# A Fourier filter ahead of a mixture of experts: corner turns on TensorE instead of through DRAM, and the imaginary sum of each product on GpSimd

## The chip, the core and the metric

The kernel runs on one core of one Trainium2 chip. The metric is the device time of one execution in microseconds (us). Less is better. The engines are TensorE (PE; its weight loads are PEld), VectorE (DVE), ScalarE (ACT), GpSimd (POOL) and SyncE (SP), which here only issues DMAs.

## What is computed

```python
batch, seq, dim = (8, 3072, 256)
X = np.fft.rfft(x, axis=1)                       # x: 8 x 3072 x 256
y = np.fft.irfft(X * (filt_r + 1j * filt_i)[None], n=3072, axis=1)
x = y.reshape(24576, 256)                        # tokens
logits = x @ w_gate                              # 8 experts
expert_idx = np.argmax(logits, axis=1)           # top 1; gate_w: its softmax
# each expert takes its first 768 tokens, in order; later ones are dropped
h = np.maximum(np.einsum('ecd,edf->ecf', disp, w1), 0.0)   # 256 -> 1024
y = np.einsum('ecf,efd->ecd', h, w2)                       # 1024 -> 256
out[i] = gate_w[i] * y[expert_idx[i], pos[i]]    # kept tokens; the others are 0
```

## The kernel before

**Which batches.** An expert is full after 768 tokens, so the first 2.5 batches hold all tokens that count, if the draw is not odd. The program runs batches t = 0, 1, 2 (`run(0, 0, FIRST)`), of the last one only half the tokens, and behind it 16 expert blocks of 384 tokens (`BLOCKS`). A second pass over the other batches stands behind a branch and is not taken.

**The transform of a batch** of 3072 tokens, seen as 128 x 24, goes in two matmul steps each way, and between them the data must be turned, from one index on the partitions to the other.

- `pe_a`: 12 matmuls of 512 columns with `wa` (item i), out to PSUM, copied to `t_out` by ScalarE (`act_a`), written to the DRAM scratch `zt` by `t_store` (issued by ScalarE and SyncE) and read back turned by `z_load`.
- `pe_forward(t, h)`: for each of eight groups h, 16 small matmuls of `z_in` into the PSUM tile `wide`. `dve_multiply` makes the four products with the filter `fab` (two instructions of 1024 columns into `prod`), `dve_sums` the real difference and the imaginary sum into `yy`. The one `wide` tile makes the next forward wait for both multiplies (`p_done`).
- `pe_inverse(t, j)`: 16 small matmuls of `yy` with `wbi`. `act_back` copies them to `v_out` and writes the DRAM scratch `vt`; `v_load` or `v_chunk` read it turned.
- `pe_product`: 12 matmuls of 512 columns with `wai` (6 of other shape for the half batch); `act_rows` copies them to `y`, which `y_store` writes to `y_rows` in DRAM, where experts gather from.
- For the router, `pe_turn` transposes `y` (four transposes of 128x128 for each product), `act_turned` copies, `pe_logits` multiplies with `w_gate`, `pe_raw` turns the logits back. `dve_route` makes ranks and slots in 30 small steps on VectorE (the largest ones, `hot_lo`, `hot_eq`, `hot_hi`, are one-hot matrices), and `pe_table` sums them into the table of tokens.

**Order.** Each engine has its own list, written out by hand. In the stage of batch t (`pe_stage`, 16 half steps h) TensorE also does `pe_a` of batch t + 1 and the tokens (product, turn, logits, raw) of batch t - 1, which run on into the next stage. In the last stage the order is a list of its own (`pe_last_stage`), and `pe_last` has the half batch's tokens.

**Experts.** A block is gathered by GpSimd (`pool_gather`), transposed (`pe_block_turn`), split into a high and a low part (`xh`, `xl`), multiplied (`up`, 48 matmuls; `down`, 72), each in three of the four part products. Weights are split the same way: the high part by ScalarE (`act_split`), the low part by VectorE for w1 and GpSimd for w2 (`low_split`). Their tiles lie over those of the transform.

## Time and profile before

| | |
|---|---|
| three runs | 538.6, 540.87, 543.45 us (median 540.87) |
| the profiled execution | 543.3 us, span 541.3 us |
| mean granted TensorE clock | 0.942 |
| busy: PE, DVE, ACT, POOL | 460.6, 246.9, 206.0, 202.3 us |
| DMA | 117.28 MB, mean 217 GB/s |

The span runs from the first to the last instruction. The granted clock is a share of 2.4 GHz; the other level is 1.2 GHz, and a number between them is a mix of both over the stretch. The busy time of an engine is an average over stages with different limits, so it has to be read stage by stage.

### The profile page before, as it was taken

Reading aid. Unit: us, or ns where it says so; the run is one execution under the profiler, and the core shown is the slowest. Engines: PE = TensorE matmul, PEld = TensorE weight load, DVE = VectorE, ACT = ScalarE, POOL = GpSimd, SP = SyncE. Lnnn points to the kernel's source line nnn. Section 1 sums busy time; section 2 is a strip of 40 time slices with the busy share of each in tenths; the row PEclk is TensorE's granted clock in tenths of the full one; section 3 lists DMA queues with packets and bytes.
Section 4 is the critical chain, followed back from the end, with each engine's and each line's share of the span. In section 5 each row is a group of like instructions: output and inputs, shape, how many; then the busy total and the mean of one; then the engine's idle time right before and its main releaser. Section 6 shows DMA issues by size and latency. Waiting matters only on the chain.

```text
span 541.3 us, 10327 instructions
## 1 busy us (share of the span) xinstructions
PE 460.6 (85%) x4190; PEld 368.3 (68%) x4190; DVE 246.9 (46%) x381; ACT 206.0 (38%) x362; POOL 202.3 (37%) x181
## 2 busy tenths in 40 slices
PE   5454977899789757988988998999999999998994
PEld 2112323345445424477988998999999999997994
DVE  2058235465666989578716332345412534133210
ACT  2301433455345314534135533344543436333221
POOL 0140100000000000637355788655867556684222
PEclk9958878999989977988999999999999999999998
DMA  8899897998597825999513209931099130681001
GB/s 298 298 361 413 279 380 240 316 377 275 171 339 250 281 72 151 375 409 380 192 61 106 79 11 360 377 129 40 31 332 386 54 134 30 223 316 46 30 22 44
DMA packets 63224, 117.28 MB, mean 217 GB/s; under 512 B 7632, under 2 KB 35056, under 8 KB 62656
## 3 DMA queue, kind: packets, MB, share of 16 engines
q1 hardware_dynamic: 38560, 75.77, 39.0%
q0 software_dynamic: 8864, 23.46, 12.4%
q10 hardware_dynamic: 15744, 17.31, 10.1%
q8 instruction: 35, 0.57, 0.4%
q14 instruction: 21, 0.17, 0.1%
HBM read 58.29 MB, written 58.23 MB: 215 GB/s over the span
## 4 chain that ended last, share of the span: by engine, by line
PE 58%; DVE 9%; DMA 5%; issue 5%; ACT 3%; SPq 2%; ACTq 0%; POOL 0%; POOLq 0%; DVEq 0%
PE psum L1335 23%; PE psum L1321 22%; PE psum L558 3%; PE psum L519 2%; PE psum L692 2%; PE psum L503 2%; DVE prod L832 2%; DMA w_raw<-in_w 2%; SPq L399 1%; PE psum L573 1%; DMA t_scratch<-t_out 1%; DVE hot_lo L983 1%; DMA g_in<-y_rows,token 1%; DMA u_scratch<-v_out 1%; PE psum L538 1%
## 5 line engine op out<-in xcount | busy, mean ns | idle before, releaser
L1146 DVE SCALAR_TENSOR_TENSOR hl<-psum,hh 128x384 fp32r<-128x384 f32 x128 | 69.0, 555 | 150.5 <-ACT hh L1098 113.5
L1335 PE MATMUL psum<-w2h,hh 128*128 128x256 f32 x384 | 109.8, 286 | 0.0
L1335 PE MATMUL psum<-w2h,hl 128*128 128x256 f32 x384 | 108.6, 283 | 0.0
L1335 PE MATMUL psum<-w2l,hh 128*128 128x256 f32 x384 | 108.6, 283 | 0.0
L832 DVE TENSOR_TENSOR prod<-psum,fab 128x1024 f32<-128x1024 f32 x48 | 56.5, 1219 | 90.8 <-PE psum L503 58.1
L1321 PE MATMUL psum<-xh,w1h 128*128 128x384 f32 x256 | 88.0, 344 | 9.6 <-DVE hl L1146 5.0
L1098 ACT ACTIVATE hh<-psum 128x384 fp32r<-128x384 f32 x128 | 60.7, 492 | 72.4 <-PE psum L1321 55.9
L1321 PE MATMUL psum<-xh,w1l 128*128 128x384 f32 x256 | 86.9, 339 | 0.0
L1321 PE MATMUL psum<-xl,w1h 128*128 128x384 f32 x256 | 86.8, 339 | 0.0
L1235 POOL DMA_INDIRECT out<-o_out,token x48 | 50.6, 1054 | 84.5 <-ACT o_out L1107 66.8
L1335 PEld LDWEIGHTS psum<-w2h,hh 128*128 128x128 f32 x384 | 73.6, 192 | 0.2 <-issue 0.2
L1335 PEld LDWEIGHTS psum<-w2l,hh 128*128 128x128 f32 x384 | 73.6, 192 | 0.0
L1335 PEld LDWEIGHTS psum<-w2h,hl 128*128 128x128 f32 x384 | 73.6, 192 | 0.0
L1207 POOL DMA_INDIRECT g_in<-y_rows,token x48 | 52.4, 1093 | 36.9 <-DVE token L1017 21.1
L1107 ACT ACTIVATE o_out<-psum,o_gate 128x256 f32<-128x256 f32 x48 | 22.8, 475 | 102.4 <-PE psum L1335 100.0
L1219 POOL DMA_INDIRECT o_gate<-gate_rows,token x48 | 48.7, 1014 | 23.6 <-issue 14.4
L1321 PEld LDWEIGHTS psum<-xh,w1h 128*128 128x128 f32 x256 | 49.1, 192 | 11.9 <-DVE hl L1146 6.3
L538 PE MATMUL psum<-x_in,wa 128*128 128x512 f32 x72 | 41.1, 713 | 12.9 <-DMA x_in<-in_x 5.6
L724 ACT COPY v_out<-psum 112x1024 f32<-112x1024 f32 x24 | 24.3, 1011 | 67.9 <-PE psum L519 55.9
L1321 PEld LDWEIGHTS psum<-xl,w1h 128*128 128x128 f32 x256 | 49.1, 192 | 0.0
L1321 PEld LDWEIGHTS psum<-xh,w1l 128*128 128x128 f32 x256 | 48.9, 191 | 0.0
L1198 POOL DMA_DIRECT2D gate_rows<-gate x2 | 1.1, 548 | 127.0 <-DVE carry L954 91.8
(108 smaller groups left out, 536.5 us busy)
## 6 DMA issues: line engine op xcount, KB each, us to landing
out<-zero SPq DMA_DIRECT2D x24, 1024.0 KB
w_raw<-in_w SPq DMA_DIRECT2D x14, 1024.0 KB
u_scratch<-v_out ACTq DMA_DIRECT2D x48, 192.0 KB, 3.9
z_in<-t_scratch SPq DMA_DIRECT2D x24, 256.0 KB, 4.6
x_in<-in_x POOLq DMA_DIRECT2D x12, 512.0 KB, 12.3
t_scratch<-t_out SPq DMA_DIRECT2D x15, 256.0 KB, 6.3
t_scratch<-t_out ACTq DMA_DIRECT2D x15, 256.0 KB, 6.5
x_in<-in_x SPq DMA_DIRECT2D x6, 512.0 KB, 6.3
```

Source lines behind the costliest of these rows:

```text
L538: nc.tensor.matmul(ps[i % 2][:, :], wa[:, :], x_in[:, c, 2 * h:2 * h + 2, :], start=True, stop=True).then_inc(a_done, 1)
L558: mm = nc.tensor.matmul(ps[i % 2][:, :], wai[:, :], v_home(t, c)[:, 2 * h:2 * h + 2, :], start=True, stop=True)
L724: nc.scalar.copy(v_out[0:A1 + HR, g % 2], back[0:A1 + HR]).then_inc(v_evac, 1)
L832: nc.vector.tensor_tensor(prod[:, n % 2, f], wide, fab[:, h, :, f, :].unsqueeze(2).to_broadcast([P, 2, 2, D]), ALU.mult).then_inc(p_done, 1)
L1098: nc.scalar.activation(hh[:, b % 2, f, :], ps[(2, 3, 6, 7)[f % 4]][:, 0:TOK], ACT.Relu).then_inc(hh_done, 1)
L1107: nc.scalar.activation(o_out[:, b % 2, s, :], ps[4 + (b * ST + s) % 2][:, 0:D], ACT.Copy, scale=o_gate[:, b % 4, s:s + 1]).then_inc(o_evac, 1)
L1146: nc.vector.scalar_tensor_tensor(out=hl[:, b % 2, f, :], in0=ps[(2, 3, 6, 7)[f % 4]][:, 0:TOK], scalar=0.0, in1=hh[:, b % 2, f, :].bitcast ...
L1207: nc.gpsimd.indirect_dma_start(out=g_in[:, b % 2, s, :], out_offset=None, in_=yd[0:have], in_offset=bass.IndirectOffsetOnAxis(ap=tokens_of ...
L1219: nc.gpsimd.indirect_dma_start(out=o_gate[:, b % 4, s:s + 1], out_offset=None, in_=gd[0:have], in_offset=bass.IndirectOffsetOnAxis(ap=toke ...
L1235: nc.gpsimd.indirect_dma_start(out=out, out_offset=bass.IndirectOffsetOnAxis(ap=tokens_of(r, b, s), axis=0), in_=o_out[:, b % 2, s, :], in ...
L1321: mm = nc.tensor.matmul(ps[(2, 3, 6, 7)[f % 4]][:, 0:TOK], wt[k][:, h, f * P:(f + 1) * P], xx[:, b % 2, h, :], start=(m == 0), stop=(m == 5))
L1335: mm = nc.tensor.matmul(ps[4 + (b * ST + s) % 2][:, 0:D], hx[:, b % 2, f, s * P:(s + 1) * P], wt[k][:, f, :], start=(f == 0 and m == 0), s ...
```

## The change

Nothing of the transform goes through DRAM scratch.

- `pe_a` now takes x as the stationary operand and `wa` as the moving one: four matmuls of 128 columns per item, 48 a batch. Channels come out on the partitions. ScalarE copies them to `t_in` with another order of the columns. `pe_turn_z` transposes `t_in` back, two items of four transposes for each of the eight groups, and `act_turned_z` copies to `z_in`.
- `pe_inverse` takes `prod` as the stationary operand: 32 matmuls of 96 columns on tiles of 64 x 64, in place of 16 of 256. `act_back` copies to `v_in` in two instructions.
- The logits are taken from `v_in`, ahead of the last transform, and transformed by themselves (`pe_raw`, `pe_route_in`). `pe_turn_v` transposes `v_in` for the products: 12 items a batch, in place of the turns of `y`.
- `dve_sums` makes the difference only, over `prod`, and `pool_sum` on GpSimd makes the sum. Both wait for the same release (`p_done`).
- Items of PSUM that ScalarE evicts share three banks in turn (`next_work`).
- A stage now has eight steps, and all tokens of batch t - 1 in the stage of batch t. The order of the last stage is that of the others. Expert 0's weights load in the last stage, and so do the first nine zero stores. For the first block the cast and the low split of expert 1 stand on VectorE between its evictions, and `act_split(act, r, 0, 1)` stands behind the block's turn.

```diff
-        back, wide = psum[:, 0:NQ, 0], psum[:, NQ:NQ + 2]
+        work = [psum[:, i].rearrange("p k d -> p (k d)") for i in range(WORK)]
+        back = [psum[:, i].rearrange("p k d -> p (k d)")[:, 0:DH * 4 * HR] for i in (3, 6)]
+        wide = psum[:, 4:6]
...
+        def x_load(sp, t, c, first):
+
+            if t > first + 1:
+                sp.wait_ge(ya_done, ya_before(t - 2) + 2 * c + 2)
                 sp.nop(nofuse=True)
-            v_chunk(sp, t, c)
-
...
+        def y_store(sp, t, c):
+
+            sp.wait_ge(ya_evac, ya_before(t) + 2 * c + 2)
...
+        def sp_stage(sp, t, a, tok, first):
+            for c in range(products(tok) // 2):
+                y_store(sp, tok, c)
+                if a is not None:
+                    x_load(sp, a, c, first)
 
...
             n = t * NG + j
-            pe.wait_ge(m_done, 2 * n + 2)
+            pe.wait_ge(m_done, n + 1)
+            pe.wait_ge(im_done, n + 1)
             if n >= 1:
-                pe.wait_ge(v_evac, n)
-            pe.wait_ge(t_evac, issued["a"])
-            if issued["ya"] > 0:
-                pe.wait_ge(ya_evac, issued["ya"])
-            for c in range(2):
+                pe.wait_ge(v_evac, 2 * n)
+            for h in range(DH):
                 for a in range(2):
-                    for q in range(NQ):
-                        quarter = slice(q * QR, (q + 1) * QR)
-                        mm = nc.tensor.matmul(back[part(a), q, :], wbi[quarter, j, a, c, :],
-                                              yy[quarter, n % 2, a, c, :], start=(c == 0), stop=(c == 1))
+                    for c in range(2):
+                        for low in range(2):
+                            for q in range(2):
+                                d = h * P + low * A1
+                                at = (h * 2 + a) * 2 * HR
+                                mm = nc.tensor.matmul(back[q][part(low), at:at + 2 * HR], prod[part(q), n % 2, 0, a, c, d:d + A1],
+                                                      wbi[part(q), j, a, c, :], start=(c == 0), stop=(c == 1))
             mm.then_inc(bi_done, 1)
...
-            nc.tensor.matmul(ps[i % 2][:, :], wa[:, :], x_in[:, c, 2 * h:2 * h + 2, :],
-                             start=True, stop=True).then_inc(a_done, 1)
...
+                pe.wait_ge(zt_done, 2 * NG * t)
+            k = next_work("pe")
+            free_work(pe, k)
+            for n in range(CH):
+                mm = nc.tensor.matmul(work[k][:, n * P:(n + 1) * P], x_in[:, c, n, h * P:(h + 1) * P], wa[:, :],
+                                      start=True, stop=True)
+            mm.then_inc(a_done, 1)
+            held[k] = (t_evac, t * 12 + i + 1)
...
+        def pe_turn_z(pe, t, g, r):
+            n = t * NG + g
+            if g == 0:
+                pe.wait_ge(t_evac, (t + 1) * 12)
+                pe.wait_ge(gaps_set, r + 1)
+                pe.wait_ge(sq_loaded, 16)
+            for j in range(2):
+                k = next_work("pe")
+                free_work(pe, k)
+                for i in range(2):
+                    for h in range(DH):
+                        p = GP * g + 2 * j + i
+                        mm = nc.tensor.transpose(work[k][:, (i * DH + h) * P:(i * DH + h + 1) * P],
+                                                 t_in[:, h, 2 * p:2 * p + 2].rearrange("p a r n -> p (a r n)"), ident)
+                mm.then_inc(zt_done, 1)
+                held[k] = (z_evac, 2 * n + j + 1)
+
...
+        def pe_turn_v(pe, t, i):
+            k = next_work("pe")
+            free_work(pe, k)
+            for n in range(2):
+                for h in range(DH):
+                    mm = nc.tensor.transpose(work[k][:, (n * DH + h) * P:(n * DH + h + 1) * P], v_in[:, h, 2 * i + n, :], ident)
+            mm.then_inc(vt_done, 1)
+            held[k] = (vt_evac, t * 12 + i + 1 if t != HALF else t * 12 + half_order().index(i) + 1)
...
+        def pe_stage(pe, t, r, a, tok, first):
+            for h in range(NG):
+                pe_forward(pe, t, r, h)
+                if tok is not None:
+                    if h == 0:
+                        if tok > first:
+                            pe_table(pe, tok - 1, 7)
+                        pe_logits(pe, tok, 0)
+                        pe_logits(pe, tok, 1)
+                    for i in turned_at(h):
+                        pe_turn_v(pe, tok, i)
+                    if h == 0:
+                        pe_raw(pe, tok)
+                    if h == 1:
+                        pe_route_in(pe, tok)
+                    if h == RANK_STEP:
+                        pe_rank(pe, tok, 7)
+                if h + ZB < NG:
+                    pe_turn_z(pe, t, h + ZB, r)
+                if h > 0:
+                    pe_inverse(pe, t, h - 1)
+                if tok is not None:
+                    for i in products_at(tok, h):
+                        pe_product(pe, tok, i)
+                if a is not None:
+                    for i in first_at(tok is not None, h):
+                        pe_a(pe, a, i, first)
+            if a is not None:
+                pe_turn_z(pe, a, 0, r)
+                pe_turn_z(pe, a, 1, r)
             pe_inverse(pe, t, NG - 1)
-
...
         def pe_last(pe, t, r):
-            pe.wait_ge(v_evac, (t + 1) * NG)
+            pe_table(pe, t - 1, 7)
+            pe_logits(pe, t, 0)
+            pe_logits(pe, t, 1)
+            for k, i in enumerate(half_order() if t == HALF else range(N2 // 2)):
+                pe_turn_v(pe, t, i)
+                if k == 3:
+                    pe_raw(pe, t)
+                if k == 7:
+                    pe_route_in(pe, t)
+            for i in range(products(t)):
+                pe_product(pe, t, i)
+            for k in range(WORK):
+                free_work(pe, k)
...
-            if h == 0 and t > 0:
-                act.wait_ge(t_written[c % 3], n * 32)
+            k = next_work("act")
             act.wait_ge(a_done, t * 12 + i + 1)
-            nc.scalar.copy(buf[:, c % 3, 2 * h:2 * h + 2, :],
-                           ps[i % 2][:, :].rearrange("p (n d) -> p n d", d=D)).then_inc(t_evac, 1)
-            if h == 1:
-                t_store(act, t, c, 0)
+            nc.scalar.copy(t_in[:, h, :, :, c * CH:(c + 1) * CH],
+                           work[k].rearrange("p (n r u) -> p u r n", n=CH, r=2)).then_inc(t_evac, 1)
+
+        def act_turned_z(act, t, g):
+            n = t * NG + g
+            for j in range(2):
+                k = next_work("act")
+                if n >= ZB:
+                    act.wait_ge(b_done, n - ZB + 1)
+                act.wait_ge(zt_done, 2 * n + j + 1)
+                nc.scalar.copy(z_in[:, n % ZB, 2 * j:2 * j + 2, :], work[k].rearrange("p (n d) -> p n d", d=D)).then_inc(z_evac, 1)
 
         def act_back(act, t, g):
-            n = t * 4 + g // 2
-            if n > 0:
-                act.wait_ge(v_written[g % 2], n * 32)
-            act.wait_ge(bi_done, t * NG + g + 1)
-            nc.scalar.copy(v_out[0:A1 + HR, g % 2], back[0:A1 + HR]).then_inc(v_evac, 1)
-            act.wait_ge(v_evac, t * NG + g + 1)
-            for a in range(2):
-                dst = vt[t, a, g * GP:(g + 1) * GP].rearrange("p q d -> q p d")
-                act.dma_start(dst, v_out[part(a), g % 2]).then_inc(v_written[g % 2], 16)
+            for q in range(2):
+                act.wait_ge(bi_done, t * NG + g + 1)
+                u = 16 * g + 8 * q
+                nc.scalar.copy(v_in[:, :, :, u:u + 8], back[q].rearrange("p (h x n) -> p h n x", h=DH, n=N2)).then_inc(v_evac, 1)
+
...
         def act_exp(act, t):
...
@@ -827,7 +710,7 @@
                 dve.wait_ge(tables[h // 2], (r + 1) * 16 * TABLE_DMAS)
             dve.wait_ge(b_done, n + 1)
             if n >= 2:
-                dve.wait_ge(m_done, 2 * n - 2)
+                dve.wait_ge(bi_done, n - 1)
             for f in range(2):
                 nc.vector.tensor_tensor(prod[:, n % 2, f], wide,
                                         fab[:, h, :, f, :].unsqueeze(2).to_broadcast([P, 2, 2, D]), ALU.mult).then_inc(p_done, 1)
@@ -835,58 +718,42 @@
         def dve_sums(dve, t, h):
             n = t * NG + h
             dve.wait_ge(p_done, 2 * n + 2)
-            if n >= 2:
-                dve.wait_ge(bi_done, n - 1)
-            nc.vector.tensor_tensor(yy[:, n % 2, :, 0, :], prod[:, n % 2, 0, :, 0, :], prod[:, n % 2, 1, :, 1, :],
+            nc.vector.tensor_tensor(prod[:, n % 2, 0, :, 0, :], prod[:, n % 2, 0, :, 0, :], prod[:, n % 2, 1, :, 1, :],
                                     ALU.subtract).then_inc(m_done, 1)
-            nc.vector.tensor_tensor(yy[:, n % 2, :, 1, :], prod[:, n % 2, 0, :, 1, :], prod[:, n % 2, 1, :, 0, :],
-                                    ALU.add).then_inc(m_done, 1)
...
+        def pool_sum(pool, t, h):
+            n = t * NG + h
+            pool.wait_ge(p_done, 2 * n + 2)
+            nc.gpsimd.tensor_tensor(prod[:, n % 2, 0, :, 1, :], prod[:, n % 2, 0, :, 1, :], prod[:, n % 2, 1, :, 0, :],
+                                    ALU.add).then_inc(im_done, 1)
...
             ex = r * E + e
-            if e > 1:
+            if e == 0:
+
+                sp.wait_ge(zt_done, 2 * NG * (FIRST if r == 0 else NB))
+                sp.nop(nofuse=True)
+            elif e == 1:
+
+                sp.wait_ge(bi_done, NG * (FIRST if r == 0 else NB))
+                sp.nop(nofuse=True)
+            else:
...
             if r == 0:
-                route(0, 4)
                 for f in range(FT):
                     upped(0, f)
                     route(FIRST_ROUTE[f], FIRST_ROUTE[f + 1])
+                    if f == 1:
+                        dve.wait_ge(w_loaded[0], (r * (E - 1) + 1) * 16)
+                        nc.vector.tensor_copy(w1h[1][:, :, :].rearrange("p h f -> p (h f)"), raw_of(1, 0)).then_inc(w1h_done, 1)
+                    if f == 4:
+                        low_split(dve, r, 1, 0)
```

On TensorE, in the stage of batch 1, one step that multiplies tokens. Before, in a step of the second stage (forward, product, turn, raw, product, turn, logits, inverse):

```order
L503 MATMUL psum<-z_in,wf 32x256 [waits p_done,tables3,z_loaded2]
L503 MATMUL psum<-z_in,wf 32x256 x15
L558 MATMUL psum<-v_in,wai 128x512 [waits ya_evac,v_evac,v_loaded1]
L573 MATMUL psum<-sq,y 128x128 [waits yt_evac,ya_evac]
L573 MATMUL psum<-sq,y 128x128 x3
L596 MATMUL psum<-nums,lg_t 128x32 [waits lg_evac]
L558 MATMUL psum<-v_in,wai 128x512 [waits ya_evac,v_evac]
L573 MATMUL psum<-sq,y 128x128 [waits yt_evac,ya_evac]
L573 MATMUL psum<-sq,y 128x128 x3
L588 MATMUL psum<-y_t,wgs 32x128 [waits lg_evac,yt_evac]
L588 MATMUL psum<-y_t,wgs 32x128 x7
L519 MATMUL psum<-yy,wbi 48x256 [waits t_evac,ya_evac,v_evac,m_done]
```

In the changed kernel, step 3 of the same stage (forward, two turns of z, inverse and four products):

```order
L403 MATMUL psum<-z_in,wf 32x256 [waits p_done,z_evac]
L403 MATMUL psum<-z_in,wf 32x256 x15
L450 MATMUL psum<-sq,t_in 128x128 [waits ya_evac]
L450 MATMUL psum<-sq,t_in 128x128 x3
L450 MATMUL psum<-sq,t_in 128x128 [waits ya_evac]
L450 MATMUL psum<-sq,t_in 128x128 x3
L420 MATMUL psum<-wbi,prod 64x96 [waits v_evac,im_done,m_done]
L420 MATMUL psum<-wbi,prod 64x96 x31
L509 MATMUL psum<-x_in,wai 128x512 [waits ya_evac,vt_evac]
L509 MATMUL psum<-x_in,wai 128x512 [waits z_evac,vt_evac] x2
L509 MATMUL psum<-x_in,wai 128x512 [waits ya_evac,vt_evac]
```

A step now holds one inverse of 32 short matmuls, two items of turns that did not exist, and all four products in a row; no wait for a DMA is left in it.

On VectorE, a step in which the routing runs. Before, in the last stage (multiplies, difference, sum, then four of the one-hot matrices' instructions):

```order
L832 TENSOR_TENSOR prod<-psum,fab 128x1024 [waits m_done,b_done,tables2]
L832 TENSOR_TENSOR prod<-psum,fab 128x1024
L840 TENSOR_TENSOR yy<-prod 128x2x256 [waits bi_done,p_done]
L842 TENSOR_TENSOR yy<-prod 128x2x256
L983 TENSOR_TENSOR hot_lo<-small,nums 128x1024 [waits route_step] x2
L986 TENSOR_TENSOR hot_eq<-small,nums 128x1152 [waits route_step]
L989 TENSOR_TENSOR hot_hi<-hot_eq,nums 128x24x48 [waits route_step]
L992 TENSOR_TENSOR hot_hi<-hot_eq,nums 128x24x48 [waits route_step]
```

In the changed kernel, step 5 and the head of step 6 of the stage of batch 1:

```order
L715 TENSOR_TENSOR prod<-psum,fab 128x1024 [waits bi_done,b_done]
L715 TENSOR_TENSOR prod<-psum,fab 128x1024
L721 TENSOR_TENSOR prod<-prod 128x2x256 [waits p_done]
L833 TENSOR_TENSOR lg<-lg 128x192 [waits route_step]
L835 TENSOR_REDUCE small<-lg 128x24 [waits route_step]
L838 TENSOR_SCALAR small<-small 128x24 [waits route_step]
L840 TENSOR_SCALAR small<-small 128x24 [waits route_step]
L842 TENSOR_SCALAR small<-small 128x24 [waits route_step]
L844 SCALAR_TENSOR_TENSOR small<-small 128x24 [waits route_step]
L849 TENSOR_TENSOR hot_lo<-small,nums 128x1024 [waits route_step] x2
L715 TENSOR_TENSOR prod<-psum,fab 128x1024 [waits bi_done,b_done,tables3]
```

The imaginary sum (L842) is gone from VectorE, and a routing step follows right behind the difference (L721). It is now on GpSimd, which had a few DMA issues there before:

```order
L727 ISA
L727 TENSOR_TENSOR prod<-prod 128x2x256 [waits p_done] x13
L1078 DMA gate_rows<-gate 128x24 [waits route_step]
L727 TENSOR_TENSOR prod<-prod 128x2x256 [waits p_done] x11
L1078 DMA gate_rows<-gate 128x24 [waits route_step]
L1087 DMA g_in<-y_rows,token_75 128x256 [waits y_stored1,y_stored2,y_stored0,gate_stored,tokens_set,set_up,b_done]
```

Twenty-four sums, one for each group of the three batches, stand ahead of the gathers, each behind its own `p_done`.

## Rows read from the trace of the kernel before

**Rows 1.** Windows by stage: stretch, its length, busy us (instructions) of each engine, clock, DMA.

```profile
30.00:86.00 56.00, 36.70 (x536) 15.10 (x536) 29.19 (x32) 13.98 (x19) 6.84 (x13) 0.77 0.98 356
86.00:142.00 56.00, 50.28 (x700) 24.47 (x692) 29.20 (x32) 28.61 (x48) 0.00 (x0) 0.97 0.87 292
142.00:206.00 64.00, 47.09 (x764) 26.07 (x748) 49.21 (x82) 24.03 (x42) 1.10 (x2) 0.92 0.67 218
...
300.00:541.00 241.00, 230.04 (x1653) 227.55 (x1651) 74.53 (x125) 93.33 (x173) 144.16 (x119) 0.99 0.41 147
```

**Rows 2.** Timeline from 129 us: start, length, engine, line, instructions, idle before.

```profile
129.34 1.10 PE L558 MATMUL psum<-v_in,wai 128*128 128x512 f32 x2 [0.25 <-issue]
...
130.27 0.60 PE L573 MATMUL psum<-sq,y 128*128 128x128 f32 x4
...
130.71 0.31 PE L596 MATMUL psum<-nums,lg_t 128*128 128x32 f32 x2
...
130.85 1.10 PE L558 MATMUL psum<-v_in,wai 128*128 128x512 f32 x2
...
132.32 0.64 PE L588 MATMUL psum<-y_t,wgs 128*32 128x128 f32 x16
...
132.89 0.64 PEld L519 LDWEIGHTS psum<-yy,wbi 32*48 32x48 f32 x32 [0.20 <-issue]
132.89 1.10 PE L519 MATMUL psum<-yy,wbi 32*48 32x256 f32 x32
...
133.93 1.09 PE L503 MATMUL psum<-z_in,wf 64*32 64x256 f32 x32
...
135.27 1.10 PE L558 MATMUL psum<-v_in,wai 128*128 128x512 f32 x2 [0.25 <-issue]
```

**Rows 3.** Groups of instructions by line, shapes apart: count, busy us, mean ns, idle before.

```profile
L832 DVE TENSOR_TENSOR prod<-psum,fab 128x1024 f32<-128x1024 f32 x48 | 56.5, 1219 | 90.8 <-PE psum L503 58.1 <-issue 32.6
...
L1069 POOL TENSOR_TENSOR w2l<-w_raw,w2h 128x2048 fp32r<-128x2048 f32 x7 | 32.3, 4614 | 2.0 <-ACT w2h L1061 1.8
...
L840 DVE TENSOR_TENSOR yy<-prod 128x512 f32<-128x512 f32 x24 | 16.6, 692 | 0.8
...
L1069 DVE TENSOR_TENSOR w1l<-w_raw,w1h 128x2048 fp32r<-128x2048 f32 x7 | 16.0, 2292 | 7.1 <-ACT w1h L1059 5.8 <-issue 1.2
```

**Rows 4.** Timelines of GpSimd and VectorE, and line L963 by itself (ns min/median/max).

```profile
247.89 4.57 POOL L1069 TENSOR_TENSOR w2l<-w_raw,w2h 128x2048 fp32r<-128x2048 f32 x1 [1.83 <-ACT w2h L1061]
...
226.81 3.48 DVE L886 CAST w1h<-w_raw 128x2048 fp32r<-128x2048 f32 x1 [5.30 <-DMA w_raw<-in_w]
...
248.23 0.56 DVE L1146 SCALAR_TENSOR_TENSOR hl<-psum,hh 128x384 fp32r<-128x384 f32 x1 [1.46 <-ACT hh L1098]
...
L963 DVE TENSOR_TENSOR lg<-lg x3: 358/359/3972, 171.4 to 248.7; 128x192 f32<-128x192 f32 x3
```

**Rows 5.** Waits of TensorE from 25 to 234 us, the longest in total.

```profile
PE psum L503 <- DMA z_in<-t_scratch: 12.8, 2, 9.9
```

**Rows 6.** Timeline of VectorE near the end of the last stage.

```profile
206.54 0.36 DVE L967 TENSOR_TENSOR lg<-lg 128x192 f32<-128x192 f32 x1
...
208.43 3.74 DVE L983 TENSOR_TENSOR hot_lo<-small,nums 128x1024 bf16<-128x1024 f32 x3
212.21 1.36 DVE L986 TENSOR_TENSOR hot_eq<-small,nums 128x1152 bf16<-128x1152 f32 x1
```

**Rows 7.** Timelines of the start, of two copies, and of the first expert matmul.

```profile
20.12 0.58 ACT L714 COPY v_in<-psum 128x512 f32<-128x512 f32 x1 [0.27 <-PE psum L538]
...
29.96 1.96 PE L503 MATMUL psum<-z_in,wf 64*32 64x256 f32 x32 [9.87 <-DMA z_in<-t_scratch]
...
100.04 1.07 ACT L714 COPY t_out<-psum 128x512 f32<-128x512 f32 x2 [1.65 <-DMA t_scratch<-t_out]
...
233.70 0.66 PE L1321 MATMUL psum<-xh,w1h 128*128 128x384 f32 x1 [1.54 <-DVE xl L895]
```

**Rows 8.** Timeline at 153 us, where the clock is at its lower level.

```profile
153.22 1.06 PE L573 MATMUL psum<-sq,y 128*128 128x128 f32 x4
```

717 lines of the change are left out of this document (250 added, 467 removed).

## The prediction

> **What bounds the kernel now.** I read the stretches first, with their cuts where one batch's inverse transforms end and the next batch's begin [rows 1]. The three transform stages take 56, 56 and 64 us, the first expert block starts at 233.7 us [rows 7], and from 300 us on TensorE is full, so about 234 us of the 541.3 us span are open to this change. In the first stage DMA is busy 98% of the time at a granted clock of 0.77: the longest wait of TensorE between 25 and 234 us is for z_in, 12.8 us in two waits [rows 5]. In the second stage the clock is 0.97 and one step, product to product, is 5.93 us of TensorE work without a gap worth naming [rows 2]: there TensorE is the bound already. In the third VectorE is busy 49.2 of 64 us [rows 1]. So the DRAM turns cost most in stage 0, at the start (last eviction of x ends at 20.7 us, first forward at 29.96 [rows 7]), and between the last inverse and the last tokens.
>
> **Prices.** At the full clock (2.4 GHz), from start to start: product of 512 columns 0.93 us, four transposes 0.44, a pair of the small raw matmuls 0.14, 16 logit records 0.57, an inverse 1.04, a forward 1.34 before a product and about 1.1 alone [rows 2]. ScalarE copies 512 columns in 0.53 when two follow each other (two in 1.07 [rows 7]). VectorE multiplies a group in 2.36 (two of 1219 ns counted with their overlap), a sum is 0.69 [rows 3].
>
> **What the change does to each, per batch.** (1) The first transform: 48 matmuls of 128 columns in place of 12 of 512: the same columns, each with a new 128x128 stationary. Two raw records, each with a 128x128 stationary, take 0.14 us, or 0.07 each, less than the 0.11 us that 128 columns in two passes take, so the load hides: 0.94 an item, as now. Bounds 0.93 and 1.2. (2) 64 new transposes as 16 items: 0.44 on TensorE, 0.53 on ScalarE, so 0.53 each through three banks. The 48 transposes before the logits become the 48 that turn v back; no difference. (3) The inverse: 64 records of 96 columns instead of 32 of 256. By columns over four tiles it is 64 x 80 ns / 4 = 1.28 us; by the records of the logits (36 ns each) 2.3. I take 1.6, nearer to the first, since weights of this kind go in at 20 ns apiece (32 in 0.64 us, row L519 of PEld) [rows 2]. (4) On GpSimd a sum of 512 columns: 4614 ns for 2048 makes 1.15 us [rows 3]; bounds 1.15 and 1.5. (5) Off ScalarE: 28 DMA issues of a batch. On: 16 copies for z and smaller ones for v, some 37 us per batch, under TensorE's load everywhere. (6) All writes and loads of scratch go, 4 x 3.1 MB a batch, 38 of the 117 MB.
>
> **The sum on GpSimd is not beside VectorE's.** While GpSimd worked on w2l from 247.89 to 252.46, a VectorE instruction with both inputs in SBUF (L963) that takes 359 ns elsewhere took 3972, and ended with it; one that reads PSUM and SBUF (L1146) took its usual 0.56 in the middle of it [rows 4]. VectorE's difference and GpSimd's sum both read prod twice, at the same release. So the difference and the sum run one after the other, 0.69 + 1.15 = 1.84 against 1.37 before, and whichever VectorE instruction with two SBUF inputs follows, a routing step in stages 1 and 2, waits 1.15. The multiplies, from PSUM, don't. (They have a new wait too, for inverse h - 2, since prod is now its operand; in TensorE's list that inverse stands ahead of the forward that they wait for anyway, so it costs nothing unless the inverse itself is late.)
>
> **Stages.** *Start*: evictions end at 20.7 as now, eight turn items 4.3, wake-ups 0.3: first forward at 25.3, 4.7 us earlier. *Stage 0*: four steps at the pace of forward, multiply, forward (1.1 + 2.36 and two wake-ups, 3.75 us; TensorE has 1.1 + 1.1 + 1.6 in it) = 15.0; four steps of 1.1 + 1.6 + 3 x 0.94 = 5.5, together 22.1; tail of eight turn items, an inverse and 0.6 of waits = 6.4. Sum 43.5, ends at 68.8 (before 86). *Stage 1*: step 0 is 1.1 + logits 3.4 (96 records of 36 ns) + six turns 3.2 + raw 1.0 + two turns 1.1 = 9.8; step 1 1.1 + 3.2 + 0.9 + 1.1 + 1.6 = 7.9; steps 2 and 3 1.1 + 1.1 + 1.6 + four products 3.8 = 7.6 each; step 4 7.1. That is 40.0. In steps 5 and 6 the route is on VectorE: 2.36 + 0.69 + 1.15 + 4.4 (six steps from 206.54 to 208.43, 1.9, and two hot_lo of 1.25) = 8.6, and 2.36 + 0.69 + 1.15 + 4.0 (one hot_lo, hot_eq 1.36, hot_hi the same) = 8.2 [rows 6], against 6.5 of TensorE, so VectorE bounds; step 7 6.5, tail 6.4. Sum 69.7, ends at 138.5 (before 142: what was won is nearly spent, since the second stage now holds all the tokens of its batch and 16 turns more). SyncE's loads of x for batch 2 now stand behind the stores of y and wait for the products that free their chunks; the last chunk comes free at the end of step 4 and is asked for in step 7, 17 us later, so I cost this at nothing (if a landing took longer, stage 1 would grow by the excess). *Stage 2*: 41.1 with the table, then 8.6 + 8.2 and a last group of 7.3: 65.2, ends at 203.7 (before 206). *Last tokens*: evictions 1.3, logits 3.4, twelve turns 6.4, raw and route 1.5, six half products 6.1 (0.93 and a switch each), block turn to first expert matmul 3.5: 22.2. Thin steps ahead of it leave the clock at half, as now at 153 us, where four transposes take 1.06 for 0.60 [rows 8]: +3. Hence 228.9 without any wait that I didn't name. The same reckoning gives 50.4 for stage 1 of before, which took 56; most of that was DMA, but I add 2 us to each of three stages: **234.9 for the first expert matmul, against 233.7**. Where the DRAM's 12.8 us and the start's 4.7 went: into 48 x 0.53 = 25 us of turns for z, 24 x 0.56 = 13 us of longer inverses, and the queued VectorE.
>
> **Into the experts.** Weights for expert 0 come earlier, and the first zeros (9 MB) go out in stage 2 and not at 220 to 240 us; neither is waited for long now. But two things move into the first block. The cast and low split for expert 1 (1.1 + 2.29 us [rows 3]; for the cast I take half of the split, which reads twice as much; its bounds are that and the 3.48 it took at 226.81 [rows 4]) are now queued on VectorE between the hl of block 0; behind them wait hl, and so TensorE's banks. And the w2l of expert 0, whose cast ScalarE now makes after the block turn, holds GpSimd 4.6 us during block 0, where routing steps of the half batch stand on VectorE and hl behind them. Block 0 and 1 have some slack now; I count 3 us (bounds 0 and 8: all of the 3.4 and 4.6). The route of the half batch, for which block 2 waits, moves with it.
>
> Sum: +1.2 + 3 = +4.2 on the span of 541.3; the profiled execution (543.3) is 2.4 above the median of 540.87, and the difference goes on the median: **545 us**, 0.8% more.
>
> **Rivals.** *A, faster: TensorE was the cheap part.* If the inverse is at its lower bound (24 x 0.3 = 7 us), GpSimd's sum is dodged by order in steps 5 and 6 (4 x 1.15 = 4.6) and no nameless waits come (6), 545 - 18 = 527. For it: the steady step of [rows 2] is packed without a gap, and there are no more queues of DMAs. Against it: in the stages bound by VectorE only part of it is seen.
> *B, slower: short records.* If the inverse goes at the logits' 36 ns (0.7 x 24 = 17 us) less the slack of stage 0's first steps (about 2), 545 + 15 = 560. It decides from about 1.8 us per inverse on. For it: no row has 96 columns.
> *C, slower: the turns run at the half clock.* The same four transposes took 1.06 us at the half clock, 0.60 at full with their tail [rows 2, 8]. Runs of transposes alone (start, two tails, head of stages 1, 2 and last, some 60 items) would then be TensorE-bound at 0.88 in place of 0.53: +21, 566. In this trace transposes stand in the middle of other matmuls, so it can't exclude it. The Trainium skill (TensorE: Matmul & The Clock Gate, Part 4: PE-mode transpose) says that transposes do not count as busy for the clock; by that rule this rival is what happens, and by the mixed steps of the rows it isn't shown.
> *D, slower: strided evictions.* The copies into t_in and v_in read PSUM across 128 or 48 elements. No row of ScalarE does so. At twice the price 36 items go from 0.94 to about 1.15 and the back copies eat the rest of the slack: +12, 557. The Trainium skill (SBUF — State Buffer, Door 1: The DMA port swizzle) puts PSUM's lines at 8 bytes and calls other patterns slow for matmuls; it gives no price for ScalarE.
>
> **Chances.** Forecast 0.42 (538 to 552), A 0.27, B 0.14, C 0.09, D 0.08. The range leaves out A's lower part and C's end: 524 to 566. A measurement here tells about 1% (5.4 us) from nothing. Faster than that: A, 0.28. Within: some two thirds of the forecast and bits of its neighbours, 0.32. Slower: the rest, 0.40.
>
> **What would show it.** First forward near 25 us, first expert matmul near 235; the inverse at 1.6 us a group; GpSimd's sums at 1.15 and routing steps of 0.36 us that take 1.5 beside them; stage 0 shorter by 12, stage 1 longer by 13, ScalarE never the releaser for long. I am wrong if the clock in stages 0 and 1 is below 0.9, if GpSimd's sum costs over 1.5, or if evictions of t_in pass 0.9 us.

## The result, and the profile after

The changed kernel takes 523.8 us (median of 4 runs) where the kernel before took 539.7 beside it: ratio 0.969, 95% interval 0.964 to 0.975. I had said 545. The profiled execution has a span of 523.0 us. Its windows, cut as before [rows 1] at the first forward of each stage, at the table product and at the first expert matmul:

```profile
23.00:68.20 45.20, 40.55 (x931) 33.19 (x931) 24.38 (x24) 22.24 (x45) 14.23 (x8) 1.00 0.35 134
68.20:130.10 61.90, 60.97 (x1115) 46.77 (x1114) 45.26 (x54) 36.81 (x73) 14.97 (x9) 1.00 0.32 104
130.10:192.30 62.20, 51.07 (x1011) 36.96 (x1010) 46.52 (x58) 27.58 (x53) 14.74 (x9) 0.88 0.58 214
192.30:214.00 21.70, 18.48 (x218) 13.41 (x214) 5.62 (x14) 13.44 (x26) 6.07 (x6) 0.96 0.81 262
214.00:523.00 309.00, 289.62 (x2038) 286.66 (x2038) 119.55 (x199) 120.41 (x221) 181.56 (x148) 0.98 0.38 133
```

In the second stage (stage 1, counted from 0) TensorE is busy for 60.97 of 61.90 us at the full clock. The DMA share of the first stage has fallen from 98% to 35%. Against the prediction, in us:

| | before | predicted | after | after less predicted |
|---|---|---|---|---|
| start, to the first forward | 30.0 | 25.3 | 23.0 | -2.3 |
| stage 0 | 56 | 43.5 | 45.2 | +1.7 |
| stage 1 | 56 | 69.7 | 61.9 | -7.8 |
| stage 2 | 64 | 65.2 | 62.2 | -3.0 |
| last tokens, with the clock | 27.7 | 25.2 | 21.7 | -3.5 |
| waits without a name | | 6 | 0 | -6 |
| from the first expert matmul to the end | 307.6 | 310.6 | 308.95 | -1.65 |

So at the first expert matmul the kernel is 19.65 us ahead of before (214.05 for 233.70 [rows 7]) and gives 1.35 back behind it. That last figure is within what repeats: in c1_changed_again, the same kernel once more, the part from the first expert matmul on takes 307.4 us and not 308.95. The steps of TensorE's stage 1, from its timeline (answers to [rows 2]):

```profile
110.91 1.09 PE L403 MATMUL psum<-z_in,wf 64*32 64x256 f32 x32
111.93 1.55 PE L420 MATMUL psum<-wbi,prod 64*64 64x96 f32 x64
113.41 3.84 PE L433 MATMUL psum<-wa,x_in 128*128 128x128 f32 x32
117.18 1.09 PE L403 MATMUL psum<-z_in,wf 64*32 64x256 f32 x32
118.53 1.55 PE L420 MATMUL psum<-wbi,prod 64*64 64x96 f32 x64 [0.25 <-issue]
120.01 3.84 PE L433 MATMUL psum<-wa,x_in 128*128 128x128 f32 x32
124.52 2.04 PE L450 MATMUL psum<-sq,t_in 128*128 128x128 f32 x16 [0.68 <-ACT t_in L602]
126.52 1.55 PE L420 MATMUL psum<-wbi,prod 64*64 64x96 f32 x64
```

A step (forward to forward) is 6.27 us, the inverse takes 1.48 from start to start, four first-transform items 3.77, and four turn items in a row (16 transposes) 2.04 with their tail. VectorE in the same steps, and GpSimd beside it:

```profile
105.83 2.35 DVE L715 TENSOR_TENSOR prod<-psum,fab 128x1024 f32<-128x1024 f32 x2 [0.16 <-PE psum L403]
108.22 0.69 DVE L721 TENSOR_TENSOR prod<-prod 128x512 f32<-128x512 f32 x1
108.83 1.43 DVE L833 TENSOR_TENSOR lg<-lg 128x192 f32<-128x192 f32 x1
...
114.22 2.35 DVE L715 TENSOR_TENSOR prod<-psum,fab 128x1024 f32<-128x1024 f32 x2
...
122.21 2.35 DVE L715 TENSOR_TENSOR prod<-psum,fab 128x1024 f32<-128x1024 f32 x2
124.60 0.69 DVE L721 TENSOR_TENSOR prod<-prod 128x512 f32<-128x512 f32 x1
```

```profile
108.28 1.77 POOL L727 TENSOR_TENSOR prod<-prod 128x512 f32<-128x512 f32 x1 [3.11 <-DVE prod L715]
...
124.64 1.78 POOL L727 TENSOR_TENSOR prod<-prod 128x512 f32<-128x512 f32 x1 [6.21 <-DVE prod L715]
```

From multiply to multiply VectorE takes 8.39 and 7.99 us, as predicted (8.6, 8.2), yet TensorE goes on at 6.27. GpSimd's sum starts 0.06 us after the start of the difference (L721) and ends 1.14 us after its end, so the 1.77 us that its row shows hold a wait. Behind the difference L833, a routing step with two inputs in SBUF, takes 1.43 us, and 0.34 where GpSimd has no sum: the two engines take turns, as [rows 4] had it. VectorE falls behind here without TensorE waiting: multiply 6 (at 114.22) starts 2.2 us after the end of its forward, and multiply 7 (at 122.21) 4.0 us after its own. The groups by line (answers to [rows 3]), and TensorE's waits from 20 to 240 us (to [rows 5]):

```profile
L727 POOL TENSOR_TENSOR prod<-prod 128x512 f32<-128x512 f32 x24 | 42.7, 1777 | 144.6 <-DVE prod L715 144.6
L420 PE MATMUL psum<-wbi,prod 64*64 64x96 f32 x1536 | 41.1, 259 | 8.5 <-POOL prod L727 5.4 <-issue 3.1
...
L612 ACT COPY z_in<-psum 128x512 f32<-128x512 f32 x48 | 25.2, 603 | 11.6 <-PE psum L450 11.4
L602 ACT COPY t_in<-psum 128x512 f32<-128x512 f32 x36 | 21.0, 586 | 9.8 <-PE psum L433 9.8
```

```profile
PE psum L403 <- DVE prod L715: 6.8, 3, 3.9
PE psum L420 <- POOL prod L727: 5.4, 1, 5.4
PE psum L420 <- issue: 3.1, 4, 1.3
PE psum L520 <- DVE lg L805: 2.5, 1, 2.5
```

The long waits (3.9 and 5.4 us) are at the end of stage 2, where TensorE has no other work and VectorE makes the one-hot matrices (answers to [rows 6]):

```profile
179.76 1.96 PE L403 MATMUL psum<-z_in,wf 64*32 64x256 f32 x32 [3.93 <-DVE prod L715]
180.26 2.29 DVE L849 TENSOR_TENSOR hot_lo<-small,nums 128x1024 bf16<-128x1024 f32 x1
...
189.54 2.84 PE L420 MATMUL psum<-wbi,prod 64*64 64x96 f32 x64 [5.36 <-POOL prod L727]
```

### The profile page after: what moved, and what is told of

Same layout as the page of the kernel before. It is cut to its first block, busy times and chain, and to the rows that moved or that the text cites. A ratio compares the mean times of both kernels' runs of the same rounds, so it can differ in the third digit from the quotient of the medians.

```text
span 523.0 us, 12605 instructions
## 1 busy us (share of the span) xinstructions
PE 477.5 (91%) x5432; PEld 433.1 (83%) x5432; DVE 243.8 (47%) x355; ACT 231.9 (44%) x434; POOL 231.8 (44%) x184
## 4 chain that ended last, share of the span: by engine, by line
PE 78%; issue 6%; DVE 6%; POOL 3%; DMA 3%; ACT 1%; POOLq 0%; SPq 0%; ACTq 0%; DVEq 0%
PE psum L1201 22%; PE psum L1215 20%; PE psum L433 7%; PE psum L420 6%; PE psum L450 4%; PE psum L403 4%; PE psum L509 4%; PE psum L474 3%; PE psum L578 2%; PE psum L464 2%; DVE prod L715 1%; DMA w_raw<-in_w 1%; POOL o_gate L1099 1%; PE psum L505 1%; DVE hot_lo L849 1%
## 5 line engine op out<-in xcount | busy, mean ns | idle before, releaser
L727 POOL TENSOR_TENSOR prod<-prod 128x512 f32<-128x512 f32 x24 | 42.7, 1777 | 144.6 <-DVE prod L715 144.6
L972 ACT ACTIVATE hh<-psum 128x384 fp32r<-128x384 f32 x128 | 61.9, 492 | 67.9 <-PE psum L1201 66.9
L1087 POOL DMA_INDIRECT g_in<-y_rows,token x48 | 49.7, 1036 | 24.8 <-issue 19.5
L1099 POOL DMA_INDIRECT o_gate<-gate_rows,token x48 | 50.1, 1045 | 23.4 <-issue 14.4
L420 PEld LDWEIGHTS psum<-wbi,prod 64*64 64x64 f32 x1536 | 36.3, 143 | 15.4 <-issue 15.4
L420 PE MATMUL psum<-wbi,prod 64*64 64x96 f32 x1536 | 41.1, 259 | 8.5 <-POOL prod L727 5.4
```

The costliest lines, as they stand in the source:

```text
L420: mm = nc.tensor.matmul(back[q][part(low), at:at + 2 * HR], prod[part(q), n % 2, 0, a, c, d:d + A1], wbi[part(q), j, a, c, :], start=(c == ...
L727: nc.gpsimd.tensor_tensor(prod[:, n % 2, 0, :, 1, :], prod[:, n % 2, 0, :, 1, :], prod[:, n % 2, 1, :, 0, :], ALU.add).then_inc(im_done, 1)
L972: nc.scalar.activation(hh[:, b % 2, f, :], ps[(2, 3, 6, 7)[f % 4]][:, 0:TOK], ACT.Relu).then_inc(hh_done, 1)
L1087: nc.gpsimd.indirect_dma_start(out=g_in[:, b % 2, s, :], out_offset=None, in_=yd[0:have], in_offset=bass.IndirectOffsetOnAxis(ap=tokens_of ...
L1099: nc.gpsimd.indirect_dma_start(out=o_gate[:, b % 4, s:s + 1], out_offset=None, in_=gd[0:have], in_offset=bass.IndirectOffsetOnAxis(ap=toke ...
```

## Experiments

Each series ran on one chip with the kernel before beside it, and the ratio is to that one. The kernel before had medians of 538.0 us beside c1, a6, a7 and a8, of 540.0 beside b1, a1, a2 and a3 and beside a9 and a10, and of 543.3 beside a4 and a5, so across series the ratios are to be compared and not the microseconds. The changed kernel run once more (c1_changed_again) is the measure of what repeats.

| run | us | ratio, 95% interval |
|---|---|---|
| c1_changed_again | 522.8 | 0.969, 0.963 to 0.974 |
| b1_sum_on_pool | 545.9 | 1.011, 1.007 to 1.014 |
| a1_sum_on_dve | 522.1 | 0.965, 0.959 to 0.971 |
| a2_route_early | 518.5 | 0.960, 0.956 to 0.964 |
| a3_turn_twice | 539.0 | 0.998, 0.996 to 1.001 |
| a4_warm | 530.5 | 0.973, 0.965 to 0.981 |
| a5_all | 529.1 | 0.972, 0.965 to 0.978 |
| a6_sum_route | 517.7 | 0.959, 0.954 to 0.965 |
| a7_small_warm | 522.3 | 0.965, 0.958 to 0.973 |
| a8_more_vector | 527.8 | 0.980, 0.975 to 0.985 |
| a9_warm_late_zeros | 517.7 | 0.958, 0.952 to 0.964 |
| a10_late_zeros | 516.2 | 0.954, 0.949 to 0.960 |

> The changed kernel itself, once more, so that the other three of this series stand beside it on the same chip. Expected: ratio 0.965 to 0.975 to the kernel before, as it had (0.9694).

### What the parts are worth, from the kernel before

```diff
-            if g == 0:
-                for i in range(3):
-                    sp.wait_ge(t_written[i], (t + 1) * 64)
...
-                sp.dma_start(z_in[to, n % ZB], zt[t, rows_, g * GP * D:(g + 1) * GP * D]
+                sp.dma_start(z_in[to, n % ZB], xt[t][rows_, g * GP * D:(g + 1) * GP * D]
...
-                t_stores(sp, first, 0, NCH)
...
+                t_stores(sp, first, 0, NCH)
```

The last two lines move SyncE's stores of the first batch behind its first loads.

> The kernel before with the first corner turn's loads (z_in) taken from the input x instead of the scratch tensor, of the same size and shape, and not waiting for the scratch stores; the stores are still made. The transform along the second axis is so made of the wrong numbers, and the routing of the tokens is another. This takes away the latency and the wait of the first turn through DRAM and none of its traffic. Theory 1 (latency: store, wait, load): the first forward comes at 21 to 23 us instead of 30 and the 12.8 us of waits for z_in go, stage 0 is 5 us shorter: 10 to 14 us faster, ratio 0.975 to 0.98. Theory 2 (traffic: DMA is 98% busy in stage 0, and the same bytes still move): the first forward is early, but stage 0 ends within 3 us of where it did: 0 to 4 us faster.

```diff
-            eng.wait_ge(t_evac, t * 12 + 2 * c + 2)
-            dst = zt[t, at:at + 2 * CH].rearrange("(n r) (p d) -> (r p) n d", r=2, d=D)
-            eng.dma_start(dst, buf[a:P:2, c % 3]).then_inc(t_written[c % 3], 16)
+            return
...
-            if h == 0 and t > 0:
-                act.wait_ge(t_written[c % 3], n * 32)
...
-                for i in range(3):
-                    pool.wait_ge(t_written[i], (first + 1) * 64)
+                pool.wait_ge(t_evac, (first + 1) * 12)
```

> As the last, and the stores of the first corner turn are left out too (12 stores of 0.26 MB a batch); the waits for them are replaced by waits for the evictions. So 9.4 MB less are written, the loads remain. Theory 2 (traffic) has this one faster than the last by 5 to 10 us (9.4 MB at 356 GB/s is 26 us of DMA time, of which stage 0's third and the start count fully), ratio 0.97 to 0.98. Theory 1 (latency) has it within 2 us of the last. Either way what both together leave to the changed kernel's 0.969 is what the second corner turn is worth.

With the wrong numbers the tokens crowded on few experts and the second pass ran (1316 and 1267 us in all), so only the traces up to the first expert matmul count. First forwards of stages 0, 1, 2, and the first expert matmul:

| | stage 0 | stage 1 | stage 2 | experts |
|---|---|---|---|---|
| before | 29.96 | 86.11 | 142.25 | 233.70 |
| loads early | 19.32 | 80.94 | 136.91 | 228.99 |
| and no stores | 18.10 | 66.42 | 120.63 | 214.00 |
| changed | 23.01 | 68.19 | 130.12 | 214.05 |

With the loads early, stage 0 starts 10.6 us earlier and half of that is lost again, since the third forward then waits for its tables:

```profile
PE psum L502 <- DMA wbi<-in_wbi: 11.6, 1, 11.6
```

That wait is not traffic alone. GpSimd issues these tables, and in the kernel before and in b2_z_early it first waits for the stores of the first batch to land. Without the stores it issues them 8.8 us earlier (first row with the stores, second row without), and the wait for `wbi` is 2.9 us:

```profile
28.29 0.73 POOL L325 DMA_DIRECT2D wf<-in_wf  x1 [27.83 <-DMA t_scratch<-v_in]
19.46 0.73 POOL L325 DMA_DIRECT2D wf<-in_wf  x1 [19.01 <-ACT v_in L708]
```

Taking the stores away as well wins another 14.5 us at the start of stage 1. So neither theory stands alone: in this order, 5.2 us come from loading early and 14.5 from the stores, that is from their bytes together with all that waits for them to land (GpSimd's tables, ScalarE's copies). These two runs don't tell bytes from waits within the 14.5.

The sum of both, 19.7 us, is also what the changed kernel is ahead by at its first expert matmul, but the two are not made of the same things. The changed kernel removes the second corner turn too, whose worth no run shows by itself, and pays for turns on TensorE. Against this last kernel it has +1.8 us at the start of stage 1, +7.7 in stage 1, -3.4 in stage 2 (62.2 for 65.6) and -6.1 in the last tokens (21.7 for 27.8), which add up to nothing.

```diff
-            nc.vector.tensor_tensor(yy[:, n % 2, :, 1, :], prod[:, n % 2, 0, :, 1, :], prod[:, n % 2, 1, :, 0, :],
-                                    ALU.add).then_inc(m_done, 1)
...
+            nc.gpsimd.tensor_tensor(yy[:, n % 2, :, 1, :], prod[:, n % 2, 0, :, 1, :], prod[:, n % 2, 1, :, 0, :],
+                                    ALU.add).then_inc(im_done, 1)
```

> The kernel before with one part of the change alone: the imaginary sum of each product goes to GpSimd, into yy as before; corner turns stay through DRAM. Theory (serialised with VectorE's difference, and in stages that wait for DMA or TensorE): first two stages unchanged, third stage (VectorE busy 49 of 64 us) loses 24 short VectorE instructions of 0.69 in all stages but gains waits of 1.13 in their place: 0 to 3 us slower, ratio 1.000 to 1.006. Rival (GpSimd takes work off VectorE and the third stage gains it): 8 x 0.69 = 4 to 6 us faster, ratio 0.99.

Slower by 1.1% (6.0 us): the theory's direction, at twice the upper end of its 0 to 3 us, and the rival is refuted. Stages 0 and 1 together are unchanged (stage 2 starts at 142.17 for 142.25). In stage 2 the last inverse starts at 208.62 for 204.81, 3.8 us later, and the last tokens add 1.1. In VectorE's timeline the routing behind a sum is held:

```profile
181.25 0.69 DVE L842 TENSOR_TENSOR yy<-prod 128x512 f32<-128x512 f32 x1
181.86 3.55 DVE L991 TENSOR_TENSOR hot_lo<-small,nums 128x1024 bf16<-128x1024 f32 x2
```

Two hot_lo of 1.23 us each take 3.55, 1.1 us more than both. By itself, in this kernel, moving the sum to GpSimd loses.

### Who sets the pace of the changed kernel

```diff
+                if t == 0:
+                    nc.vector.tensor_tensor(hot_eq[:, :, :], hi.unsqueeze(2).to_broadcast([P, N2, NHI]),
+                                            hi_numbers.unsqueeze(1).to_broadcast([P, N2, NHI]), ALU.is_equal)
```

> The changed kernel with hot_eq written three extra times on VectorE in the second stage, twice in its step 5 and once in its step 6 (1.36 us each, 4.1 in all; it is written again with its real value later). My prediction had taken VectorE's pace (8.6 and 8.2 us) for the pace of these two steps; the trace of the changed kernel has VectorE at 8.4 and 8.0 and TensorE at 6.3 and 6.3. Theory 1 (VectorE may fall behind by about one step, since TensorE needs its product only a step later; the two long steps used that up just when the stage ended, where the inverse started 0.1 us after its product): the second stage grows by 3 to 4.1 us. Theory 2 (there is more room than that, or the end of the stage is bound by something else): it grows by under 1 us.

Stage 1 takes 65.7 us for 61.9 (3.8 more for 4.1 added), and the whole kernel 4.9 us more than the changed kernel in this series. Theory 1 holds, and the timeline of TensorE shows where:

```profile
119.08 1.76 PE L403 MATMUL psum<-z_in,wf 64*32 64x256 f32 x32 [1.99 <-DVE prod L715]
120.88 2.45 PE L420 MATMUL psum<-wbi,prod 64*64 64x96 f32 x64
```

Forward 7 needs multiply 6 to be done. In the changed kernel multiply 6 ends at 116.57 and forward 7 starts at 117.18: 0.6 us of room. Multiply 7 and its two sums are done at 126.42, and inverse 7 starts at 126.52: 0.1 us of room. What VectorE is behind by lies under the 3.84 us of `pe_a` and the turns, which stand between forward 7 and inverse 7.

```diff
-EXP_STEP = 3
-RANK_STEP = 4
+EXP_STEP = 2
+RANK_STEP = 3
...
-STEPS_BY = [0, 2, 4, 8, 16, 24, 27, 28]
+STEPS_BY = [0, 4, 10, 18, 24, 26, 27, 28]
```

> The changed kernel with the routing steps of a batch spread earlier over the steps of a stage (0, 4, 10, 18, 24, 26, 27, 28 done by the end of each step, where it was 0, 2, 4, 8, 16, 24, 27, 28) and the exponential and the rank products one step earlier. Theory: in the third stage TensorE waits 3.9 and 5.4 us for VectorE in steps 5 to 7, because there the routing is longer than TensorE's work; moved ahead into steps in which TensorE has logits, turns and products, it hides. Third stage 4 to 6 us shorter (58 for 62.2), second stage unchanged (61.9), total 518 to 520. Rival 1 (the waits only move: the steps now laden become bound by VectorE): second and third stage both 2 to 4 us longer, 526 to 530. Rival 2 (the idle stretch was filled by the clock: the thin tail ran at half clock and still does): within 1 us of 523.8.

518.5 us. Stage 1 is 61.5 us (61.9 in the changed kernel), stage 2 58.9 (62.2), and the three waits at its end are 2.4, 1.95 and 2.6 us for 1.1, 3.9 and 5.4. As expected, stage 1 is set by TensorE and the end of stage 2 by VectorE.

```diff
...
-            nc.gpsimd.tensor_tensor(prod[:, n % 2, 0, :, 1, :], prod[:, n % 2, 0, :, 1, :], prod[:, n % 2, 1, :, 0, :],
+            nc.vector.tensor_tensor(prod[:, n % 2, 0, :, 1, :], prod[:, n % 2, 0, :, 1, :], prod[:, n % 2, 1, :, 0, :],
...
-                        pool_sum(pool, t, h)
```

> The changed kernel (523.8 us) with the imaginary sum back on VectorE, right behind the real difference; nothing else differs. Theory (the two sums run one after the other, whichever engines they are on, since the trace of the changed kernel has the sum ending 1.78 us after the difference starts): VectorE needs 0.69 + 0.69 = 1.38 us, the inverse is released 0.4 us earlier, and no routing instruction behind them is held up by GpSimd's 1.13 us. In the stages bound by TensorE nothing is gained; in the third stage up to 4 steps win 0.4 each. Expected 0 to 2 us faster, 522 to 524. Rival (the split relieves VectorE, and that is part of the 17 us gained): 24 x 0.69 us more on VectorE, of which the third stage's 8 steps and the two steps before it show: 3 to 6 us slower, 527 to 530.

The ratio of 0.965 can't be told from 0.969. The trace shows a difference where VectorE bounds: the step from multiply to multiply that took 7.99 us takes 7.51, and stage 2 ends 1.5 us sooner. VectorE's timeline at 176 us in it:

```profile
176.37 2.35 DVE L715 TENSOR_TENSOR prod<-psum,fab 128x1024 f32<-128x1024 f32 x2
178.75 0.69 DVE L721 TENSOR_TENSOR prod<-prod 128x512 f32<-128x512 f32 x1
179.36 0.68 DVE L723 TENSOR_TENSOR prod<-prod 128x512 f32<-128x512 f32 x1
179.96 1.22 DVE L845 TENSOR_TENSOR hot_lo<-small,nums 128x1024 bf16<-128x1024 f32 x1
```

The rival (3 to 6 us slower) is refuted: in this kernel, splitting the sums between the two engines saves nothing.

> The changed kernel with the imaginary sum back on VectorE and the routing steps spread earlier, without any unused matmuls. Theory: their single gains (1.7 and 5.3 us against 523.8) add in part, since the wait for the last product of the third stage (2.6 us left with the early routing) falls by the 0.4 us a step that the sums end sooner: 0.4 to 2 us faster than early routing alone, 4.5 to 7 us faster than the changed kernel in this series. Rival (both relieve the same wait): equal to early routing alone, 4 to 5 us faster than the changed kernel.

Both together: 517.7 us, with stage 2 at 56.2 us for 62.2 of the changed kernel in this series. By ratio that is 0.959, and 0.960 for early routing alone, which is within the noise; the shorter stage 2 (56.2 for 58.9) is from the traces.

```diff
-                for i in range(2):
+                for i in (0, 1, 0, 1):
```

> The changed kernel with each of the two transposes of every z item and half issued twice in a row, so that the 16 items of a batch cost TensorE 0.44 us more each and nothing more on ScalarE. Theory (TensorE bounds the start only in part and the stages nearly throughout): of 16 x 3 x 0.44 = 21 us the sixteen items at the start and the two tails hide some under ScalarE's 0.53 an item; 12 to 18 us slower, 536 to 542. Rival (the turns are covered by VectorE's pace of 3.75 us a step, or by ScalarE): under 6 us slower.

15.3 us slower than the changed kernel. The start and stage 2 hold 8 items each and grow by 3.5 us each, all of the 3.5 that the added transposes cost there. Stages 0 and 1 hold 16 each (7.0 us added) and grow by 4.6 and 6.7; the last tokens are 1.6 shorter. So the turns are on the path nearly everywhere, except in part of stage 0, and TensorE sets the time of the changed kernel's transform up to the last steps of stage 2. At the start this kernel has 64 transposes in a row, at a granted clock of 1.00:

```profile
19.34 7.21 PE L450 MATMUL psum<-sq,t_in 128*128 128x128 f32 x64 [0.68 <-ACT t_in L602]
```

### The clock, and a stop in TensorE's list

```diff
+                if r == 0 and a is None and h >= 5:
+                    free_work(pe, 0)
+                    for _ in range((6, 10, 12)[h - 5]):
+                        nc.tensor.matmul(work[0][:, 0:3 * P], ident, sq[:, :, :], start=True, stop=True)
```

> The changed kernel (523.8 us) with 6, 10 and 12 unused matmuls of 384 columns put ahead of the inverse in steps 5, 6 and 7 of the third stage, where TensorE idles 3.9 and 5.4 us and its records run at the half clock (an inverse 2.6 us for 1.5, the table product 1.96 for about 1.0). Theory: the clock stays up, and what runs slow now (two inverses, a forward, the table, the first logits, in all some 5 us of excess) is given back where it isn't hidden by VectorE: 2 to 4 us faster, 520 to 522. Rival 1 (the stretch is set by VectorE, and the slow records only fill its gaps): within 1 us. Rival 2 (the unused matmuls delay the inverse more than the clock gives back): 2 to 5 us slower.

> The changed kernel with the imaginary sum back on VectorE, the routing steps spread earlier, and the unused matmuls of the third stage's last steps, all three. By themselves the first two gave 522.1 and 518.5 where the changed kernel has 523.8. If their gains are of different waits they add: 516 to 517, and with the clock held 513 to 516. Rival (VectorE is the bound of the third stage's end in both, so that what one gives the other can't, and the unused matmuls now stand in the way): 518 to 521.

The traces show rival 2 of the first in both. The records run at the full clock (the inverse 1.55 us, the table product 1.20), but the filling takes 4.14, 6.72 and 8.01 us, more than the gaps: stage 2 is 65.2 and 65.1 us, where the kernels without the filling have 62.2 and 56.2. By the times alone only the second is told from its kernel without the filling (0.972 for 0.959); the first (0.973 for 0.969) isn't.

> The last one with 2, 3 and 3 unused matmuls of 384 columns (0.67 us each) in the third stage's steps 5 to 7, where TensorE would wait 1 to 2.6 us. With 6, 10 and 12 the records there ran at the full clock but the filling itself took 18.9 us and the stage grew by 4.4. Theory: eight matmuls take 5.4 us, fit into the waits and hold the clock: 1 to 3 us faster than the last. Rival (so few don't hold the clock, or the stage is set by VectorE): within 1 us of the last.

The filling (1.56, 2.20, 2.20 us) now fits, stage 2 is 55.7 us for 56.2, and the clock is 1.00 up to 190 us. Yet the kernel comes out no faster (522.3 for 517.7, with intervals that overlap). The timeline shows a reason:

```profile
184.23 1.55 PE L420 MATMUL psum<-wbi,prod 64*64 64x96 f32 x64 [0.98 <-DVE prod L725]
185.72 1.20 PE L532 MATMUL psum<-hot_hi,hot_lo 128*128 128x96 bf16 x24
186.84 1.06 PE L464 MATMUL psum<-v_in,wgs 128*32 128x128 f32 x26
191.50 3.47 PE L464 MATMUL psum<-v_in,wgs 128*32 128x128 f32 x70 [3.59 <-issue]
```

TensorE stops for 3.59 us in the middle of a run of logits that waits for no semaphore. In the changed kernel the same run stops after 42 records for 0.99 us; here, with 16 records more ahead, after 26. So the stop is at a fixed place in the list. a6_sum_route, which gets there 2.3 us later, stops for 1.55 us.

The trace of the DMA queues shows what comes late. In the 1 us from 189 to 190 us it has this row:

```profile
q8 instruction: 1, 0.02, 5.5%
```

It is one packet of 16 KB on a queue named `instruction`. It starts at 189.0 and ends at 189.9, and TensorE goes on at 191.50. In all six kernels that stop in these logits (the changed one, a1, a2, a6, a7 and a8, for 0.6 to 3.6 us) such a packet ends 1.5 to 1.6 us before TensorE goes on: in the changed kernel it ends at 195.15 and TensorE goes on at 196.68.

```diff
+        def sp_last(sp, t, r):
+            raw_load(sp, r, 1, 0)
+            raw_load(sp, r, 1, 1)
+            for c in range(products(t) // 2):
+                y_store(sp, t, c)
             if r == 0:
                 sp.wait_ge(zero_set, 1)
...
                 for k in range(FIRST_ZEROS):
                     sp.dma_start(out_z[k], zero_view).then_inc(first_zeroed, 16)
-
-        def sp_last(sp, t, r):
-            raw_load(sp, r, 1, 0)
-            raw_load(sp, r, 1, 1)
-            for c in range(products(t) // 2):
-                y_store(sp, t, c)
```

The zero stores stood at the end of the last stage's list and now stand behind the last stores of y.

> As the kernel with early routing, the sum on VectorE and the 2, 3 and 3 unused matmuls, but the nine 1 MB stores of zeros are issued behind the last stores of y (from about 208 us) and no longer in the third stage's end. There the last inverse ran at 184.2 us at the full clock, the logits then stopped after 26 of 96 records for 3.6 us that no semaphore explains, and the first expert matmul came at 210.9. In the kernels without unused matmuls (16 records) the stop is after 42 records, so it is at a fixed place in TensorE's list. Theory (the engine's instructions are loaded by DMA and come late while the zero stores hold the DMA at its limit): without the stores the stop goes, last inverse to first expert matmul falls from 26.7 to 21 to 23 us, and the whole is 1 to 4 us faster unless the zeros now delay the first gathers. Rival (the stop has nothing to do with DMA traffic): it stays at over 3 us.

> The same move of the zero stores without the unused matmuls (early routing and the sum on VectorE alone). Its stop is 1.55 us long behind record 42 and the logits ahead of it run partly at the half clock. Theory: the stop goes, 1 to 2 us faster than with the zeros in the third stage (517.7, ratio 0.9591). Rival (the zeros behind the y stores collide with the gathers of the first blocks): 2 to 6 us slower.

```profile
184.00 1.55 PE L420 MATMUL psum<-wbi,prod 64*64 64x96 f32 x64 [1.18 <-DVE prod L725]
185.49 1.19 PE L532 MATMUL psum<-hot_hi,hot_lo 128*128 128x96 bf16 x24
186.61 2.83 PE L464 MATMUL psum<-v_in,wgs 128*32 128x128 f32 x96
...
205.08 0.41 PE L1201 MATMUL psum<-xh,w1h 128*128 128x384 f32 x1 [1.39 <-DVE xl L762]
```

With a DMA share of 0.29 from 180 to 190 us instead of 1.04, all 96 records go through in 2.83 us, and from the last inverse to the first expert matmul it is 21.1 us for 26.7. The instruction packet now starts at 180.8, ahead of the run. The rival of the first is refuted: the stop comes with the traffic. Without unused matmuls it is gone too (a10_late_zeros: 96 in 3.22 us). That kernel has the lowest median of the study, 516.2 us and 0.954, though 0.959 for a6_sum_route and 0.958 for a9_warm_late_zeros can't be told from it.

What holding the clock wins (2.6 us at the first expert matmul, 205.08 for 207.69) is lost again behind it: 310.2 us to the end for 307.3. The loss is in one stretch of the experts, one block long, which takes 22.9 us for 19.9 (a9_warm_late_zeros first):

```profile
300.20:323.10 22.90, 19.42 (x127) 19.07 (x127) 5.11 (x10) 7.58 (x14) 16.68 (x13) 0.93 1.04 384
303.70:323.60 19.90, 17.79 (x127) 17.44 (x127) 5.11 (x10) 7.58 (x14) 16.49 (x13) 1.00 1.04 383
```

There TensorE waits 3.5 us for hl and not 2.1, and behind the longer wait its clock is partly at the lower level (0.77 from 310 to 315 us). a7_small_warm and a6_sum_route also have a mean clock of 0.92 in this stretch, and take 22.7 and 21.4 us; a6_sum_route has no unused matmuls, so they aren't needed for it. Why hl comes later stays open.

## Why the prediction was wrong

None of the three signs that I had named for being wrong came: the clock was 1.00 in stages 0 and 1, GpSimd's sum cost 1.14 us behind the difference, and an eviction of `t_in` 0.59. The prices were near; the path was wrong.

**The failed step is stage 1 (69.7 predicted, 61.9 measured), and in it "in steps 5 and 6 the route is on VectorE ... so VectorE bounds".** The sum 2.36 + 0.69 + 1.15 + 4.4 was right (8.39 us measured for 8.6), its use was not. I charged TensorE with VectorE's time in each step. TensorE needs multiply h only for forward h + 1 and its inverse, and at the end of a stage 3.84 us of `pe_a` and the turns stand ahead of the last inverse. TensorE took 6.28 and 6.27 us, 4.3 less than the 16.8 of the prediction. a8_more_vector shows that this was about all the room there was: of 4.1 us more on VectorE, 3.8 showed.

**Steps 0 to 4 of the stages were priced too high.** 36.4 us for 40.0 in stage 1 and 37.6 for 41.1 in stage 2: the four products took 3.63 us and not 3.8, the inverse 1.48 and not 1.6, six turns in a row 2.80 and not 3.2 (0.47 each), and 96 logit records 2.76 and not 3.4 (29 ns each in a long run, where the row of 16 had given 36). Each is small; together they are some 3.5 us in each of two stages.

**"2 us of unnamed waits in each of three stages" did not exist as such.** Stage 1 had 0.9 us of waits in all, and those of stage 2 stand in the steps that were priced by VectorE. Stage 0 came out 1.7 us over its price. In its first steps TensorE stopped for 1.32 and 0.82 us in the middle of inverses, without a semaphore, and each time it went on 1.3 us behind the end of a 16 KB instruction packet (33.50 and 38.64 us). These look like the stop of the last section, though only the first came in full traffic (a DMA share of 1.02 from 31 to 36 us, 0.40 from 36 to 41). The 2 us of the prediction came from stage 1 of the kernel before, with a DMA share of 0.87 (its 56 us against a reckoning of 50.4), which was no evidence for stages with 0.32.

**The start and the last tokens.** First forward at 23.0 for 25.3: I had kept 20.7 as the end of the evictions, but the first transform now takes 12.9 us where it took 14.5, and the eight turns with their wake-ups 3.9, not 4.6. Last tokens 21.7 for 25.2: the logits and the turns again. I also had 3 us for the half clock. a10_late_zeros, without the stop in the list, takes 20.9 us there, and a9_warm_late_zeros, with the full clock too, 19.6: the clock is worth 1.3.

**Experts.** +1.35 for +3, within its bounds of 0 and 8, and no more than two traces of the same kernel differ by (1.6 us).

**Rivals.** A had 527 and 523.8 came, but its number was met partly by luck. Of its three terms, the nameless waits (6) were indeed absent. The inverse, 1.48 us for 1.6, gave 2.9 us and not 7. GpSimd's sum was not dodged by order: steps 5 and 6 gave 4.3 us by the room between the two engines. The rest of the 21 us at the first expert matmul came from the start, the logits, the turns and the last tokens, which A didn't name. B did not happen: the inverse was 1.48 us wherever the clock was full, and took 2.5 to 2.8 only at the end of stage 2, where the mean clock was 0.69. C did not happen: the 32 transposes that stand alone at the start took 3.95 us, 0.49 for four where the half clock had 1.06 [rows 8], at a clock of 1.00, and in a3_turn_twice 64 of them took 7.21 us, 0.45 for four, at 1.00 too. The Trainium skill's rule that transposes don't count as busy (TensorE: Matmul & The Clock Gate, Part 4: PE-mode transpose) had this rival happen; the trace doesn't agree. No run here has transposes alone for longer than 7.21 us. D did not happen: L602 (into `t_in`) reads PSUM with a stride and takes 586 ns, L612 without one 603; for 384 columns L618 (into `v_in`) with a stride takes 482, L625 without one 479.

## What to carry to other kernels

When another engine's steps are longer than TensorE's, don't add the difference step by step: follow which forward needs which product, and count only what is left when the buffers and the work between have been used up. Ask of a removed DRAM turn what its stores held up, not only the load that waits for them: here the stores were 14.5 of 19.7 us. And a sum moved to GpSimd beside VectorE's own two-input work freed nothing here.

## What the runs showed of the hardware

- In the run of logits TensorE stopped for 0.6 to 3.6 us at a fixed place of its list while the zero stores held the DMA share near 1 (1.04 in a7_small_warm), and didn't with 0.29. Each time it went on 1.5 to 1.6 us after a 16 KB packet of the instruction queue had ended. That this packet holds TensorE's next instructions is inferred from the times; shown is that the stop goes with the traffic. The Trainium skill (Runtime: NRT & Kernel Launch, Instruction fetch mechanics) has this loading hidden by the issue of instructions; if the packet is what it seems, it was not hidden here.
- Transposes alone kept the full clock: 32 in a row took 3.95 us in the changed kernel and 64 took 7.21 us in a3_turn_twice, both at a granted clock of 1.00 and right behind other matmuls.
- A VectorE instruction with only one tensor as input was held too: L810, a TENSOR_SCALAR on 128x24, takes 0.17 us alone and 1.25 when it stands behind a difference while GpSimd's sum runs. It started at 102.21 and ended at 103.46, and the sum ended at 103.43.

```profile
L810 DVE TENSOR_SCALAR small<-small x3: 168/1249/1249, 102.2 to 222.0; 128x24 f32<-128x24 f32 x3
```
